# Rounding w_ch1 and the first batch's x within the last four pairs of an attention + mixer kernel

## The reference

```python
# B, H, S, D = 4, 8, 576, 64;  d_model 512, d_tok 256, d_ch 1536
q_rot, k_rot = rotate(q), rotate(k)                      # rope
attn = softmax(q_rot @ k_rot^T / sqrt(D))                # with + 1e-09 in the divisor
x    = (attn @ v) laid out as (B, S, H * D)
h    = relu(x^T @ w_tok1) @ w_tok2
u    = x + h^T
out  = u + relu(u @ w_ch1) @ w_ch2
```

## Time and profile before

| what | us |
|---|---|
| median of 3 runs | 622.94 |
| lowest, highest | 622.36, 627.05 |
| the profiled execution's own time | 621.9 |
| its span, first to last instruction | 619.9 |
| mean granted TensorE clock | 0.999 |

### The profile page before, as it was taken

One profiled execution on the slowest core, in us unless ns is written; L12 is line 12 of the kernel. 1 busy time (PEld: TensorE's weight loads), 2 busy tenths in 40 slices (PEclk: granted clock), 3 DMA queues, 4 the chain that ended last, 5 costly groups with the idle time before them and its releaser, 6 DMA issues.

```text
span 619.9 us, 19511 instructions
## 1 busy us (share of the span) xinstructions
PE 598.1 (96%) x7796; PEld 550.4 (89%) x7796; DVE 445.2 (72%) x844; ACT 387.9 (63%) x725; POOL 274.4 (44%) x240
## 2 busy tenths in 40 slices
PE   2999999999999999998999999999999999999997
PEld 1788888788888888878999999999999999999996
DVE  5678878778788888755568885389725699364895
ACT  2566667676666677753635556775557766567753
POOL 4666677776666663339000006830028600168100
PEclk9999999999999999999999999999999999999999
DMA  5335534444556552170005310000310003200002
GB/s 137 84 86 152 148 109 133 113 130 135 135 136 169 159 137 71 49 242 2 1 1 203 87 51 27 1 2 1 108 54 0 0 0 85 78 0 1 1 2 77
DMA packets 49870, 48.18 MB, mean 78 GB/s; under 512 B 12800, under 2 KB 42048, under 8 KB 49792
## 3 DMA queue, kind: packets, MB, share of 16 engines
q1 hardware_dynamic: 49488, 47.00, 26.5%
q10 hardware_dynamic: 304, 0.07, 0.1%
HBM read 30.24 MB, written 9.44 MB: 64 GB/s over the span
## 4 chain that ended last, share of the span: by engine, by line
PE 93%; DVE 2%; DMA 2%; ACT 1%; issue 0%; DVEq 0%
PE rest L632 15%; PE slot L592 11%; PE slot L1115 8%; PE slot L1117 8%; PE slot L1116 8%; PE rest L531 8%; PE rest L1115 6%; PE rest L1117 6%; PE rest L1116 6%; PE slot L588 3%; PE slot L1147 2%; PE slot L531 2%; DMA moved_q<-turned_q 2%; PE rest L1147 2%; PE rest L224 1%; PE rest L221 1%
## 5 line engine op out<-in xcount | busy, mean ns | idle before, releaser
L800 DVE TENSOR_REDUCE neg_max<-slot 128x1 f32<-128x576 f32 x144 | 106.6, 756 | 23.4 <-PE slot L592 15.8
L1106 POOL TENSOR_TENSOR w_ch_part<-w_ch_sums,w_ch_part 128x512 fp32r<-128x512 f32 x21 | 30.9, 1474 | 180.4 <-ACT w_ch_part L1357 180.4
L1421 ACT ACTIVATE pieces<-h 128x288 fp32r<-128x288 f32 x168 | 74.0, 445 | 49.5 <-PE slot L1117 25.1
L632 PE MATMUL rest<-v,pt 128*64 128x65 f32 x2880 | 101.9, 224 | 0.0
L632 PEld LDWEIGHTS rest<-v,pt 128*64 128x64 f32 x2880 | 90.7, 137 | 10.5 <-ACT pt L723 6.2
L723 ACT ACTIVATE pt<-rest 128x320 f32<-128x320 f32 x144 | 62.7, 435 | 51.8 <-PE rest L531 50.9
L809 DVE COPY pt<-rest 128x320 f32<-128x320 f32 x144 | 70.2, 487 | 33.5 <-PE rest L531 32.9
L592 PE MATMUL slot<-turned_k,turned_q 64*128 64x288 f32 x256 | 85.8, 439 | 4.7 <-DMA moved_q<-turned_q 2.4
L592 PE MATMUL slot<-moved_k,moved_q 64*128 64x288 f32 x256 | 86.1, 441 | 0.0
L1512 DVE TENSOR_TENSOR pieces<-h,pieces 128x288 fp32r<-128x288 f32 x168 | 74.8, 456 | 9.4 <-ACT pieces L1421 9.0
L714 ACT ACTIVATE prob_a<-slot,neg_max 128x576 f32<-128x576 f32 x80 | 59.3, 742 | 17.5 <-DVE neg_max L800 14.4
(11 more groups left out here) (236 smaller groups left out, 1793.4 us busy)
## 6 DMA issues: line engine op xcount, KB each, us to landing
moved_q<-turned_q SPq DMA_DIRECT2D x31, 160.0 KB, 2.7
raw_qk<-in_q_dram SPq DMA_DIRECT2D x16, 256.0 KB, 2.6
raw_v<-in_v_dram SPq DMA_DIRECT2D x16, 256.0 KB, 3.0
x_scratch<-x_pair SPq DMA_DIRECT2D x16, 256.0 KB, 2.7
stage_or_x<-x_scratch SPq DMA_DIRECT2D x16, 256.0 KB, 4.1
raw_qk<-in_k_dram SPq DMA_DIRECT2D x15, 256.0 KB, 2.9
w_ch_whole<-in_moe_w_ch_dram SPq DMA_DIRECT2D x8, 384.0 KB, 3.4
w_ch_A_whole<-in_moe_w_ch_dram SPq DMA_DIRECT2D x4, 768.0 KB, 8.0
```

What stands on the lines that cost most here:

```text
L632: mm = pe.matmul(to[cols], pt_of(p, i)[:, j, cols], w, start=(j == 0), stop=(j == G), skip_group_check=True)
L800: dve.tensor_reduce(neg_max[p % 2][:, i:i + 1], score_slot(p, i)[:, :, 0:HALF], AX.XY, ALU.max, negate=True).then_inc(maxed, 1)
L1421: act.activation(pieces[:, ring(m), 0, :], source[WEIGHTS[n]][:, ft, :], ACT.Copy).then_inc(piece_hi, 1)
```

## The change

prob_a gets a place of its own (in what was spare memory), so that hi's blocks 2 and 3 are free during attention; the DMAs that later overwrite that memory wait for the fifth turn of the last pair. w_ch1 hi is rounded in pairs 12, 13, 14 and 15 (the last half behind them), w_ch1 lo all by POOL. x hi: tiles 0 and 1 in pair 14, 2 and 3 in pair 15, the last behind it; x lo: 0 to 3 by POOL, the last by DVE. At attention's end PE does the first product ahead of turn 7, and all products ahead of the last two `values`; DVE's last guard, invert and normalise come behind the mixer's first step.

```diff
-        with ExitStack() as placed:
-            sb(placed, "w_ch1_first", [P, CT // 2, CH])
-            prob_a = sb(placed, "prob_a", [P, CT // 2 * CH])
...
-    sb(ctx, "spare_too", [P, 4576])
+    sb(ctx, "spare_too", [P, 4576 - NG * S])
+    prob_a = sb(ctx, "prob_a", [P, NG * S])
...
     def gpsimd(pool):
...
-            if p == N - 1:
-                token.split_lo(pool, 0, 0)
-                token.split_lo(pool, 0, 1)
+            if p >= N - 2:
+                for t in range(2):
+                    token.split_lo(pool, 0, 2 * (p - (N - 2)) + t)
             if 3 <= p < 3 + len(PIECES):
                 weights_lo(p - 3)
-            if N - 2 <= p < N:
-                w1.split_lo(pool, p - (N - 2))
+            if p > N - CT:
+                w1.split_lo(pool, p - (N - CT) - 1)
+        w1.split_lo(pool, CT - 1)
...
     def tensor(pe):
...
         first, p = slot[0], N
+        pe.wait_ge(exped, N * TILES - 1)
+        token.products(pe, 0, 0, first).then_inc(token.x_used, 1)
         turn(p - 1, 7)
         values(p - 1, 5)
         values(p - 1, 6)
-        pe.wait_ge(exped, N * TILES - 1)
-        token.products(pe, 0, 0, first).then_inc(token.x_used, 1)
         token.products(pe, 0, 1, first).then_inc(token.x_used, 1)
         turn(p - 1, 8)
-        values(p - 1, 7)
-        values(p - 1, 8)
         token.products(pe, 0, 2, first).then_inc(token.x_used, 1)
         token.products(pe, 0, 3, first).then_inc(token.x_used, 1)
         token.products(pe, 0, 4, first).then_inc(token.sums_ready, 1)
+        values(p - 1, 7)
+        values(p - 1, 8)
...
     def scalar(act, h1_of_batch_0):
...
             copy_up(p - 1, 8)
-            if N - 3 <= p < N - 1:
-                w1.split_hi(act, p - (N - 3), 0)
-            if p == N - 1:
-                act.wait_ge(products, 4 * N)
-                token.split_hi(act, 0, 0)
+            if p >= N - CT:
+                w1.split_hi(act, p - (N - CT), 0)
             exponent(p, 2)
...
             copy_up(p, 3)
+            if p == N - 2:
+                act.wait_ge(products, 4 * N)
+                token.split_hi(act, 0, 0)
+            if p == N - 1:
+                token.split_hi(act, 0, 2)
             exponent(p, 5)
             exponent(p, 6)
             copy_q(p + 1)
+            if p == N - 1:
+                token.split_hi(act, 0, 3)
             copy_up(p, 4)
             exponent(p, 7)
             copy_up(p, 5)
+            if p == N - 1:
+
+                copy_up(p, 6)
             exponent(p, 8)
...
-            if N - 3 <= p < N - 1:
-                w1.split_hi(act, p - (N - 3), 1)
-            if p == N - 1:
+            if N - CT <= p < N - 1:
+                w1.split_hi(act, p - (N - CT), 1)
+            if p == N - 2:
                 token.split_hi(act, 0, 1)
-            copy_up(p, 6)
+            if p < N - 1:
+                copy_up(p, 6)
             copy_up(p, 7)
 
         p = N
-        token.split_hi(act, 0, 2)
+        token.split_hi(act, 0, 4)
         copy_up(p - 1, 8)
-        token.split_hi(act, 0, 3)
-        token.split_hi(act, 0, 4)
-        w1.split_hi(act, 2, 0)
-        w1.split_hi(act, 2, 1)
-        w1.split_hi(act, 3, 0)
+        w1.split_hi(act, CT - 1, 1)
         act.wait_ge(token.sums_ready, 1)
         h1_of_batch_0(act)
-        w1.split_hi(act, 3, 1)
...
     def vector(dve):
...
         p = N
         copy_low(p - 1, 7)
-        normalise(p - 1, "A")
+        normalise(dve, p - 1, "A")
+
+        dve.wait_ge(token.x_lo_done, G)
+        token.split_lo(dve, 0, G)
         copy_low(p - 1, 8)
-        token.split_lo(dve, 0, 2)
-        token.split_lo(dve, 0, 3)
-        guard(p - 1, "B")
-        invert(p - 1, "B")
-        token.split_lo(dve, 0, 4)
-        normalise(p - 1, "B")
-        w1.split_lo(dve, 2)
+
+    def last_output(dve):
+        for step in (guard, invert, normalise):
+            step(dve, N - 1, "B")
...
     def buffers_left(sp):
 
         sp.wait_ge(scores, N * TILES)
+        sp.wait_ge(turned, (N - 1) * TILES + G + 1)
...
         token_lo(0, slot[0])
+        first.last_output(dve)
...
                 for c in range(CT):
                     u_lo(b, c)
-                    if c == 1:
-                        w1.split_lo(dve, 3)
```

More of the change, by code:

```diff
@@ L109, in build @@
         with ExitStack() as ctx:
-            first = attention(nc, ctx, whole, sb, slot, rest, ident, stage_or_x, raw_qk, rope_sb, rope_half, prob_a, token, wt1,
+            first = attention(nc, ctx, whole, sb, slot, rest, ident, stage_or_x, raw_qk, rope_sb, rope_half, token, wt1,
                               wt2, w1, x_stored, q, k, v, w_tok1, w_tok2, w_ch1, rope, x_scratch)
@@ L139, in _ @@
                     then.vector(dve)
-Attention = namedtuple("Attention", "sync gpsimd tensor scalar vector last_store buffers_left values_left slot_left")
+Attention = namedtuple("Attention", "sync gpsimd tensor scalar vector last_output last_store buffers_left values_left slot_left")
 Mixer = namedtuple("Mixer", "sync gpsimd tensor scalar vector first_token_hi")
@@ L225, in products, with attention @@
         return mm
-def attention(nc, ctx, whole, sb, slot, rest, ident, stage_or_x, raw_qk, rope_sb, rope_half, prob_a, token, wt1, wt2, w1, x_stored,
+def attention(nc, ctx, whole, sb, slot, rest, ident, stage_or_x, raw_qk, rope_sb, rope_half, token, wt1, wt2, w1, x_stored,
               q, k, v, w_tok1, w_tok2, w_ch1, rope, x_scratch):
@@ L763, in scalar, with guard, invert, normalise @@
                 weights_hi(p - 3)
-            if N - 3 <= p < N - 1:
-                w1.split_hi(act, p - (N - 3), 1)
-            if p == N - 1:
+            if N - CT <= p < N - 1:
+                w1.split_hi(act, p - (N - CT), 1)
+            if p == N - 2:
                 token.split_hi(act, 0, 1)
-            copy_up(p, 6)
+            if p < N - 1:
+                copy_up(p, 6)
             copy_up(p, 7)
         p = N
-        token.split_hi(act, 0, 2)
+        token.split_hi(act, 0, 4)
         copy_up(p - 1, 8)
-        token.split_hi(act, 0, 3)
-        token.split_hi(act, 0, 4)
-        w1.split_hi(act, 2, 0)
-        w1.split_hi(act, 2, 1)
-        w1.split_hi(act, 3, 0)
+        w1.split_hi(act, CT - 1, 1)
         act.wait_ge(token.sums_ready, 1)
         h1_of_batch_0(act)
-        w1.split_hi(act, 3, 1)
+    def guard(dve, p, h):
+        if no(p):
+            return
+        t0, t1 = HEADS[h]
+        dve.wait_ge(o_added, p * TILES + t1)
+        dve.tensor_tensor(guarded[p % 2][:, t0:t1], output(h)[:, :, D], eps[:, t0:t1], ALU.add).then_inc(guard_done, 1)
+    def invert(dve, p, h):
+        if no(p):
+            return
+        t0, t1 = HEADS[h]
+        dve.wait_ge(guard_done, 2 * p + "AB".index(h) + 1)
+        dve.reciprocal(inverse[p % 2][:, t0:t1], guarded[p % 2][:, t0:t1]).then_inc(inv_done, 1)
+    def normalise(dve, p, h):
+        if no(p):
+            return
+        a, (t0, t1) = "AB".index(h), HEADS[h]
+        dve.wait_ge(inv_done, 2 * p + a + 1)
+        if p > 0:
+            dve.wait_ge(x_stored, p * STORED)
+        dve.tensor_tensor(x_pair[:, 1 - a:NG, a, :], output(h)[:, :, 0:D],
+                          inverse[p % 2][:, t0:t1].unsqueeze(2).broadcast_to([P, t1 - t0, D]), ALU.mult).then_inc(x_done, 1)
     def vector(dve):
@@ L809, in copy_low @@
             dve.tensor_copy(pt_of(p, i)[:, :, low], rest[:, 1, 0:NG * D].rearrange("p (j n) -> p j n", j=NG)).then_inc(low_done, 1)
[L811 to L833, removed]
         dve.memset(raw["q"][0:TAIL, 1, G, :], 0.0).then_inc(zero_halves, 1)
@@ L855, in vector @@
             copy_low(p, 0)
-            guard(p - 1, "B")
+            guard(dve, p - 1, "B")
             copy_low(p, 1)
@@ L863, in vector @@
             copy_low(p, 3)
-            invert(p - 1, "B")
-            normalise(p - 1, "B")
+            invert(dve, p - 1, "B")
+            normalise(dve, p - 1, "B")
             copy_low(p, 4)
@@ L869, in vector @@
             copy_low(p, 5)
-            guard(p, "A")
+            guard(dve, p, "A")
             copy_low(p, 6)
-            invert(p, "A")
+            invert(dve, p, "A")
         p = N
         copy_low(p - 1, 7)
-        normalise(p - 1, "A")
+        normalise(dve, p - 1, "A")
+        dve.wait_ge(token.x_lo_done, G)
+        token.split_lo(dve, 0, G)
         copy_low(p - 1, 8)
-        token.split_lo(dve, 0, 2)
-        token.split_lo(dve, 0, 3)
-        guard(p - 1, "B")
-        invert(p - 1, "B")
-        token.split_lo(dve, 0, 4)
-        normalise(p - 1, "B")
-        w1.split_lo(dve, 2)
+    def last_output(dve):
+        for step in (guard, invert, normalise):
+            step(dve, N - 1, "B")
     def last_store(sp):
@@ L903, in attention @@
     return Attention(sync=sync, gpsimd=gpsimd, tensor=tensor, scalar=scalar, vector=vector,
-                     last_store=last_store, buffers_left=buffers_left, values_left=values_left, slot_left=slot_left)
```

(1 more changed line is left out.)

## The result

The changed kernel takes 628.09 us (median of 7 runs, 626.8 to 630.62) against 623.60 for the kernel before (7 runs, 622.36 to 627.05): ratio 1.0072, 95% interval 1.0044 to 1.0099, slower by 0.7%. The forecast was 627.7 with a range of 624.0 to 630.5. The profiled execution of the change took 627.66, its span is 625.6 us (before: 621.9 and 619.9).

The account below looks back on a forecast made before the run. PE was taken as the bound, 93% of the chain that ended last. 621.9 - 3.0 (stops) + 0.8 (ACT work) + 5.5 (wait) + 2.0 (clock) = 627.2, with 0.5 for run level 627.7; range 624.0 to 630.5.

Parts of the forecast that it names:

- The wait of pair 12: ACT's first w_ch1 rounding waits for the eighth load; PE stands 5.5 us ahead of turn 1.
- The clock: After PE's stop in pair 12 the granted clock falls to the lower level, costing 2.0 us.
- the likelier case: Pair 12's wait with the clock's fall: 627.7 us in all, chance 0.45.
- the 3.5 us at the kernel's end: Time from PE's last matmul to the clock's drop; the expected 5.4 us stop is longer, so a fall was likelier.
- rival B: Pair 12's wait comes without a clock fall: 625.7 us in all, chance 0.28.
- D: After the wait PE stays slow as long as at the start, costing 4.8: 630.5 us, chance 0.10.
- The tail: Around attention's end: stops removed give 3.0 us; added ACT work in pairs 14 and 15 costs 0.8.
- All three stops: PE's stops ahead of turn 7 (0.86 us), the first L1147 (0.87) and in hidden(0) (0.99) would go.
- (4): ACT's x roundings in pairs 14 and 15 delay PE at three places, 0 to 0.5 us each, 0.8 taken.
- a turn of 0.53 us is slow because of the stop before it: PE begins slower after each stop (0.53 against 0.47 us), so 3.0 us was taken for the tail's 2.72.
- DVE's rounding of x tile 4 meeting GpSimd's block 2: Shared SBUF port: DVE may wait up to 3.5 us, but PE asks only later; cost nothing either way.
- The offset: 0.5 us added to the sum because two earlier runs lay 0.5 and 1.0 above the profiled execution.
- Rival C: Pair 12's wait costs PE nothing because the load is early or its wait passed: 620.2 us, chance 0.05.

Follow-up runs that it names:

- e3: The kernel before with only ACT's roundings of w_ch1 blocks 0 and 1 one pair earlier (pairs 12 and 13); 630.55 us, ratio 1.0102.
- e1: The changed kernel with the eight w_ch1 loads one pair earlier in SP's program (pairs 3 to 10); 620.45 us, ratio 0.9936; run again, 620.08 us.
- e2: The changed kernel with the first w_ch1 rounding moved to the end of pair 12, behind exponent 8; 621.66 us, ratio 0.9968.
- e5: The changed kernel with each w_ch1 load ahead of the load of q in SP's program, same pair; 624.11 us, ratio 1.0019.
- t1: The kernel before with only the product of x tile 0 moved ahead of turn 7 of the last pair; 622.11 us, ratio 0.9981.
- t2: e1 with values 7 and 8 put back ahead of the last three products; 620.30 us, ratio 0.9956.
- t3: e1 with the rest of w_ch1's block 3 back on DVE, between the second and third u_lo; 619.70 us, ratio 0.9950.
- b1: e1 with q's turn ahead of values 2 in every pair and x tile 1's rounding behind tile 6's copy in pair 14; 620.89 us, ratio 0.9959.

## Why the prediction was right

**The wait of pair 12** was the largest term, and it was there as described: ACT behind the eighth load, PE ahead of turn 1, the DMA named as releaser. Forecast 5.5 us, measured 4.68 in the change and 5.25 (the stop) in e3. The profiled execution of the change accounts for 0.9 of the difference: ACT came to the rounding 1.5 us later than before (copy at 209.91 instead of 208.38) by chance and the load only 0.6 (211.62 instead of 211.02), and the wait shrinks by the difference of the two. e3 has it near full size, and e1 and e2 take it away by two different edits.

**The clock** fell, as the likelier case had it. Priced at 2.0, it cost 2.49 in the change and, from turn 1 to the next pair's k transposes, 2.14 in e3 (18.17 us against 16.03, 0.22 of it a late move of q). The reason that I gave was weaker than the outcome: I compared the stop with the 3.5 us at the kernel's end, and the fall came 2.5 us behind PE's last matmul in e3, and in one execution of e5 with a stop of only 2.40. The rival B, no fall, rested on the same comparison. The price that D took, 4.8, was from a start whose slow stretch is itself not the same each time (turn 2 at full pace before, not in the change).

**The tail** was forecast at -3.0 + 0.8 and measured at -2.67. All three stops went. The mis-sized step is the added ACT work of (4): of the three places one shows a stop, 0.25 us ahead of turn 7 in pair 14, not 0.8 us in all. That a turn of 0.53 us is slow because of the stop before it was misread: turn 1 in the earlier trace rows takes 0.53 with none. It made 3.0 out of the 2.72 that the three stops add up to; the traces have 2.9 (2.67 and the 0.25 lost), so the size was near and what the 0.2 comes from is not shown. Of the stops' causes, t1 and t2 show the first two as described; for the third the chain of waits had the right engine, and t1 and t3 add that the length came from the meeting with GpSimd, not from DVE's own 1.75.

**DVE's rounding of x tile 4 meeting GpSimd's block 2**, weighed as free either way, did not happen: GpSimd was through at 278.17 and DVE began at 279.21, 0.69 us.

**The offset**: the 0.5 us added for the level of the runs was too little for the kernel before (its median over seven runs is 623.6, 1.7 above its profiled execution) and about right for the change (0.4). That the forecast of 627.7 lies within 0.4 us of 628.09 is partly luck: the terms of the change, 5.3 us in sum, were 0.8 more than the 4.5 between the medians, and the base, 622.4, was 1.2 too low. The mechanism was not luck: e1, e2 and e3 show it.

Rival C is e1's situation, and it gave 620.45 and 620.08 where C said 620.2; by the distance to before (3.7 and 3.4 us, where C had 2.7 to the 622.94) it was a little better than C.

## What to carry to other kernels

Before an operation is moved to an earlier place in an in-order engine, look up when its inputs land, in the queue that issues them: "an earlier pair" is not free because the engine has room there, the first instruction that waits holds everything behind it. Where an early place is wanted, move the load with it. And a stop of TensorE in mid kernel is to be priced twice, once for its length and once for the half clock that may follow.

## What the runs showed that I had not expected

In the profiled execution of e5 the clock went to 1.2 GHz after a stop of PE of 2.40 us, when PE was already busy again, and stayed there for 3.4 us; after the stops of 4.56 (the change) and 5.25 us (e3) it stayed there for 6.8 us each time. Five of e5's twelve runs have a mean clock too high for such a fall. In the profile of e1, whose longest stops in mid kernel are 1.61 and 1.45 us, it did not fall. What was lost is close to half of the time in which PE worked at the lower level: 2.49 of 5.7 us in the change (217.02 to 222.7), 2.14 of 4.1 in e3 (215.51 to 219.6), 1.54 of 3.4 in e5 (17.57 us from turn 1 to the next k transposes, against 16.03). The rest of the 6.8 us fell into the stop itself, where a slow clock costs nothing more.

Much of the run to run scatter of this kernel seems to have one cause: the move of q lands with hardly any room ahead of PE's need. In the kernel before, moves go out at 154.07 and 202.31 and PE asks for them 2.9 and 2.7 us later (at 156.94, where it then stands for 1.04, and at 205.01), and a move takes 2.4 to 4.4 us to land, 2.7 in the median. So a late landing becomes a stop. The slow stretch at the start is a second part, as said. Turning q earlier (b1) removed the stops in the one profile taken and narrowed the spread of 12 runs from 5.8 to 1.4 us, at a cost of 0.1 us in most pairs and 0.35 in the two with roundings behind them.
